# Key-value moments of linear attention computed in 32-column instead of 64-column matmuls

## The reference

```
a, b = S1 @ x, S2 @ x            # 8 numbers each, per token and head
phi(x) = outer(a, b).reshape(64) # 64 features
kv[f, d] = sum_s phi(k)[s, f] * v[s, d]     # 64 x 32 per head
z[f]     = sum_s phi(k)[s, f]               # 64 per head
out      = (phi(q) @ kv) / (phi(q) . z + 1e-6)
x = RMSNorm(out), gated layer with silu: 128 -> 1536 -> 128, 4352 tokens
x = soft mixture: dispatch softmax over tokens into 32 slots, 8 experts of 4 slots, combine softmax
```

## Time and profile before

| what | us |
|---|---|
| median of 3 runs | 295.54 (294.04 to 296.53) |
| the profiled execution's own time | 296.13 |
| its span, from the first to the last instruction | 294.3 |
| PE busy in the span | 280.9 (95%) |
| PEld busy | 231.3 (79%) |
| DVE busy | 230.2 (78%) |
| ACT busy | 157.1 (53%) |
| POOL busy | 33.6 (11%) |

### The profile page before, as it was taken

How to read it: one execution, slowest core, us unless ns; L and a number is a source line. 1 busy time by engine, 2 the same in 40 slices (tenths; PEclk the granted TensorE clock), 3 DMA queues, 4 the chain that set the end, 5 groups by cost and what they waited for, 6 DMA issues and landing times.

```text
span 294.3 us, 6608 instructions
## 1 busy us (share of the span) xinstructions
PE 280.9 (95%) x2544; PEld 231.3 (79%) x2544; DVE 230.2 (78%) x443; ACT 157.1 (53%) x302; POOL 33.6 (11%) x58
## 2 busy tenths in 40 slices
PE   6889998999999999999999999999999999999990
PEld 6777876888887888888878878888788878997570
DVE  4778699957999889679988896797689688784532
ACT  2576654634666465446674653465546546556431
POOL 2279110000100100013001000100010003000000
PEclk9999999999999999999999999999999999999995
DMA  6999670227222102212221022179210322410016
GB/s 174 352 219 218 132 218 0 38 36 210 78 35 47 26 7 40 40 28 76 40 42 25 7 44 37 25 266 351 40 27 16 51 33 61 111 25 3 0 54 253
DMA packets 65393, 25.62 MB, mean 87 GB/s; under 512 B 50001, under 2 KB 62034, under 8 KB 65362
## 3 DMA queue, kind: packets, MB, share of 16 engines
q1 hardware_dynamic: 64786, 24.78, 35.4%
q10 hardware_dynamic: 576, 0.43, 0.5%
HBM read 17.45 MB, written 2.23 MB: 67 GB/s over the span
## 4 chain that ended last, share of the span: by engine, by line
PE 79%; SPq 9%; DVE 5%; DMA 2%; issue 2%; ACT 1%; DVEq 0%
PE bank L1112 77%; SPq L389 5%; DMA q_in<-in_q 2%; PE bank L1196 1%; DVE hid L943 1%; DVE area L1104 1%; SPq L395 1%; SPq L413 1%; DVE hl L954 1%; SPq L417 1%; SPq L393 1%; DVE area L829 0%; PE bank L1422 0%; ACT silu L644 0%; PE bank L1209 0%
## 5 line engine op out<-in xcount | busy, mean ns | idle before, releaser
L644 ACT ACTIVATE silu<-bank 128x512 f32<-128x512 f32 (+1 forms) x108 | 61.9, 574 | 78.7 <-PE bank L1112 77.5
L943 DVE TENSOR_TENSOR hid<-bank,silu 128x512 f32<-128x512 f32 (+1 forms) x108 | 70.7, 655 | 27.0 <-PE bank L1112 23.1
L954 DVE TENSOR_TENSOR hl<-hid,hh 128x512 fp32r<-128x512 f32 (+1 forms) x108 | 71.5, 662 | 0.1
L652 ACT ACTIVATE hh<-hid 128x512 fp32r<-128x512 f32 (+1 forms) x107 | 64.5, 603 | 4.2 <-DVE hid L943 3.8
L1112 PE MATMUL bank<-xh,wgh 128*128 128x512 f32 (+1 forms) x109 | 42.6, 391 | 0.2 <-DVE hid L943 0.2
L1112 PE MATMUL bank<-hh,woh 128*128 128x512 f32 (+1 forms) x108 | 42.5, 394 | 0.2 <-DVE hl L954 0.2
L1112 PE MATMUL bank<-xh,wgl 128*128 128x512 f32 (+1 forms) x109 | 41.2, 378 | 0.0
L1112 PE MATMUL bank<-hh,wol 128*128 128x512 f32 (+1 forms) x108 | 41.1, 380 | 0.0
L1112 PE MATMUL bank<-xh,wvl 128*128 128x512 f32 (+1 forms) x108 | 41.1, 380 | 0.0
L1112 PE MATMUL bank<-xh,wvh 128*128 128x512 f32 (+1 forms) x109 | 41.1, 377 | 0.0
L1112 PE MATMUL bank<-hl,woh 128*128 128x512 f32 (+1 forms) x108 | 41.0, 380 | 0.0
(11 more groups left out here) (158 smaller groups left out, 333.6 us busy)
## 6 DMA issues: line engine op xcount, KB each, us to landing
area<-in_moe_w SPq DMA_DIRECT2D x8, 512.0 KB, 5.5
area<-in_moe_w SPq DMA_DIRECT2D x1, 4096.0 KB, 12.8
area<-area SPq DMA_DIRECT2D x112, 32.0 KB, 2.0
q_in<-in_q SPq DMA_DIRECT2D x16, 128.0 KB, 3.4
y_nat<-in_v SPq DMA_DIRECT2D x4, 512.0 KB, 7.9
out<-area SPq DMA_DIRECT2D x8, 256.0 KB, 3.0
area<-in_k SPq DMA_DIRECT2D x14, 128.0 KB, 6.7
y_nat<-area SPq DMA_DIRECT2D x112, 16.0 KB, 1.8
```

Of the source, the lines that this page charges most:

```text
L644: act.activation(silu[n][:, 0:w], gate_b[n][:, 0:w], ACT.Silu).then_inc(s_silu_ready, 1)
L652: act.activation(hh[m % NH][:, 0:w], hid[m % 2][:, 0:w], ACT.Copy).then_inc(s_hh_ready, 1)
L943: dve.tensor_tensor(hid[n][:, 0:w], val_b[n][:, 0:w], silu[n][:, 0:w], ALU.mult).then_inc(s_hid_ready, 1)
L954: dve.tensor_tensor(hl[m % NH][:, 0:w], hid[m % 2][:, 0:w], hh[m % NH][:, 0:w].bitcast(F32), ALU.subtract).then_inc(s_hl_ready, 1)
```

## The change

Each matmul of 64 weight columns becomes two of 32 (NS = 32), by the same 33 values; the halves land in the PSUM partitions 0 to 31, 32 to 63, 64 to 95 and 96 to 127, so that a pair of heads takes four column groups of the array in turn instead of two.

```
                                 for x in range(2):
                                     h = 2 * hp + x
-                                    ins = mm(mom_b(b)[x * FT:(x + 1) * FT, hp, x * DA:(x + 1) * DA],
-                                             kp[g][:, t, h * FT:(h + 1) * FT], v_aug[:, G3 * g + t, h, :],
-                                             start=(g == 0 and t == 0), stop=(g == NG - 1 and t == G3 - 1))
+                                    for f in range(0, FT, NS):
+                                        ins = mm(mom_b(b)[x * FT + f:x * FT + f + NS, hp, x * DA:(x + 1) * DA],
+                                                 kp[g][:, t, h * FT + f:h * FT + f + NS], v_aug[:, G3 * g + t, h, :],
+                                                 start=(g == 0 and t == 0), stop=(g == NG - 1 and t == G3 - 1))
                 if NG - 1 in groups:
                     ins.then_inc(s_kmom_done, 1)
```

## The result

The changed kernel takes 296.89 us (median of 20 runs, 296.01 to 297.58) against 295.69 us for the kernel before: a ratio of 1.0042, 95% interval 1.0023 to 1.0060 (two of the 20 executions before, 352 and 555 us, are not in the ratio). The profiled execution took 296.94 us, its span is 295.1 us.

What follows compares the result with a forecast made beforehand. TensorE's own instruction stream was taken to bound the kernel from 42 to 257 us; three bursts saving 0.69 us each (2.07 us), with batch 0 counted as 0, took 295.54 to 293.47, say 293.5 us; range 292.2 to 295.9.

Steps and rivals of the forecast that it cites:

- What bounds the kernel: From 42 to 257 us TensorE's own instruction stream sets the end, busy 213.97 of 215 us; before 46 us others do.
- What a pair would cost after, and whether the queue can feed it: In the moments, 8.4 ns a pair if like the logits, 11.7 if queue-fed; burst 1.38 us, saving 0.69 us.
- The cover behind the bursts: After each burst of moments, `output` of slice 1 has its inputs ready, so no new wait for DVE takes back the saving.
- The sum over batches 1 to 3: Three later bursts of moments, each 0.69 us shorter, save 2.07 us in all.
- 11.7 ns as the pace of the queue: In a burst, TensorE's queue issues a load-and-matmul pair every 11.7 ns after the first 32 pairs at 8.4 ns.
- Batch 0: First burst, from 10.52 us: gain counted as 0, at most 0.4 us, since DVE's wait for the queries' DMA absorbs it.
- slower side: In the moments, issue becomes the bound at 27 ns a pair: three bursts add 5.4 us, 300.9 us; chance 0.09.
- The rounds are not faster: In the moments, a matmul's two records run in line, or the queue just keeps even: 295.0 to 296.6 us; chance 0.18.
- signs of being wrong: TensorE begins to wait for DVE behind a burst, or the granted clock changes with the shorter bursts; no size given.

Runs made afterwards that it cites:

- the calm start: Changed kernel with SP holding the loads of the gated layer's weights and all that follow until batch 0's moments end; profiled execution 300.05 us.

## Why the prediction was wrong, step by step

*What bounds the kernel* was right for 46 to 257 us.

*What a pair would cost after, and whether the queue can feed it,* was right in kind and size: 1.38 us from first to last record was forecast, and the three late bursts took 1.77 - 0.199 = 1.57, 1.39 and 1.57. The cover behind the bursts held: TensorE waited for no other engine there. The sum over batches 1 to 3 was 2.07 us; measured 1.73. That the size came out is in part luck: I had made it of 32 pairs at 8.4 ns, the others at 11.7, and then the middle of that and of 8.4 throughout. In the trace the starts of the three late bursts are 8.9 to 9.3 ns apart throughout, but for one or two pauses of 0.09 to 0.17 us in each, for which I have no cause. The forecast's 11.7 ns as the pace of the queue is thus not what happened. I had asked only how fast entries can be issued, and not where they come from.

*Batch 0 is the step that failed.* I counted it at 0, at best a gain of 0.4 us. It cost 3.1 us at 46 us, and 2.9 us in the kernel with nothing else changed. I had looked for what waits for the moments among the kernel's own engines and DMAs; the wait that opened was TensorE's for its own instructions. What the runs showed in its place: the store ends after 220 matmul and 220 or 221 load records, 449 instructions each time with the 9 or 8 waits and the like that the trace has for TensorE beside these records, in all five kernels that get there before 17 us, with the changed form or with idle matmuls, and the refill stands behind the input loads. In the kernel before there is no such wait, since by then TensorE was not so far: the same stretch to 12.60 us holds 145 matmul records there.

The sum that was missing compares two times. TensorE went through the last 256 of the 449 instructions from 10.57 to 12.78 us, in 2.2 us; the kernel before took from 11.09 to 20.38, 9.3 us. The refill, counted from the first of these 256, took 3.7 us with idle DMA engines (10.42 to 14.16) and 6.2 with the input loads (10.57 to 16.78). That it is asked for at that instruction is inferred, from these times and from the ones below.

*The late half of the saving* is the smaller part of the failure in the changed kernel, but it alone kept a kernel from the forecast's gain: with batch 0 left as before it took 295.77 us, not 293.5, with the same wait for instructions in its third burst. Where no burst was cut, at 293.90 and 293.96 us, the forecast's time was nearly reached. In the changed kernel the three bursts were whole, but a wait of 0.4 us for the feature transfers of block 7 opened at 214.77 us, and some 0.3 us were lost in block 2 (27.64 us of the chain from one `normalised_T` to the next instead of 27.33), for which I have no cause. Its third burst was whole although it has all the halves: with 72 more pairs ahead the pieces end at other places in it. 3.1 - 1.73 + 0.4 + 0.3 gives 2.1 us, by which TensorE's last stage is late. The span grew by 0.8 only, and the profiled time by 0.81, because the last output transfers happened to take less time in that execution; the medians differ by 1.2 us, so part of that last step stays open.

*The rivals.* None of mine was this one. The "slower side" had issue as its mechanism, but as a rate: 27 ns a pair in every burst. That is refuted, at 9.7 to 11.0 ns. "The rounds are not faster" is refuted by the same rows. The range, 292.2 to 295.9, missed by 1.0 us. One of the prediction's signs of being wrong did show: the granted clock changed, though by the standstill and not by the shorter bursts.

The Trainium skill bears on this, in "Runtime: NRT & Kernel Launch", section "Instruction fetch mechanics", which I had not weighed: instructions come by DMA in blocks of 256, the next being fetched while the current one is executed, and the section calls the cost of a boundary mostly hidden. The block agrees with this profile: each q8 packet has 16,384 bytes, and 576 more records took q8 from 20 to 22 packets. It agrees with the count of the stops too: the late one comes after 1737 matmul records, 1737 loads and 47 waits and the like, 3521 instructions, and 3521 - 449 = 3072 is twelve times 256. Hidden the boundary was not, at the two kinds of place that the runs show: at the start, where TensorE goes through 256 instructions in 2.2 us and the DMA engines are full, and where a whole block is gone through inside one dense burst.

For the second the counts and the packets bear this out. The stop came when 136 pairs of the third burst were done. The piece that ended there had begun 8 pairs into the burst, and TensorE went through its 128 pairs in about 1.2 us; the packet with the next one moved in the three stopped kernels 0.2 to 0.4 us after the start of the burst, took 1.0 to 1.5 us, and TensorE went on 1.3 to 1.4 us after its end. With 24 pairs fewer ahead, the end of the piece falls behind the burst, where a pair takes 230 ns, and there was no stop in three profiles of such kernels. It is a near thing: in the kernel with the halves for batches 1 to 3, the first burst holds some 123 of a piece's 128 pairs and does not stop. That piece begins just ahead of the burst, among the long matmuls, where the issuing side is ahead of the array (it took the wait in front of the burst at 56.96 us, the burst began at 59.59), and the packet moved at 56.52 us.

## What to carry to other kernels

Splitting matmuls into narrower column groups pays where twice the moving columns cost nothing (here the split took a pair from 29.1 to about 10 ns, at twice the pairs), but it doubles the instructions, and the store of instructions is a resource of its own: look for idle time released by "issue" in front of an instruction that has nothing to wait for, and for the same count of records ahead of it. A dense stretch of small matmuls cost nothing in the middle of long ones where no piece lay within it, 1.2 to 1.6 us where one did, and 4 us while the inputs were being loaded; where a burst must be long, shift it by a few instructions and look again. The best version found keeps batch 0 and one group of batch 1 in 64 columns and takes 293.9 us, 0.5 and 0.9% less than the kernel before in two measurements.

## What the hardware showed that I had not expected

A 4-us standstill at the start cost more than itself: the granted clock went to 0.50 for over 3 us, and the 32 records of attention took 2.03 us of merged time instead of 1.22 on the old kernel's 1.00. The clock fell at 16.97 us, just after TensorE had gone on at 16.78. The length of the stop alone does not decide it: in the profile with idle matmuls it stood for 2.22 us and the clock stayed at 1.00, in the calm start for 1.53 us and the clock fell to 0.50 from 14.2 to 17.6 us.

A matmul of 64 float32 weight columns by 33 and one by 66 moving columns cost the same (29.1 and 30.1 ns a pair), and 32 columns in four groups a third of it (9.7 to 11.0 ns).
